# Fourier transform and two feed-forward layers: part of the fold on TensorE, and other sequences of GpSimd, ScalarE and the DMA queue

## What is computed

```python
X = np.fft.fft(np.fft.fft(x, axis=1), axis=2).real      # x: 2 x 3008 x 256
rms = sqrt(mean(X*X, -1) + 1e-6);  xn = X / rms * rms_g
h = silu(xn @ w_gate) * (xn @ w_val) @ w_out            # d_ff 1536
out = (h2 * cos(h2)) @ w2_out,   h2 = h @ w_in          # d_ff 2048
```

## Time and profile before

| | us |
|---|---|
| median of 3 runs (1007.44 to 1008.67) | 1007.55 |
| the profiled execution: its time | 1008.31 |
| its span | 1006.5 |
| PE busy in the span | 985.5 (98%) |
| DVE busy | 752.1 (75%) |
| ACT busy | 636.7 (63%) |
| POOL busy | 366.1 (36%) |

### The profile page before, as it was taken

How to read it: one execution, slowest core, us unless ns; L and a number is a source line. 1 busy time by engine, 2 the same in 40 slices (tenths; PEclk the granted TensorE clock), 3 DMA queues, 4 the chain that set the end, 5 groups by cost and what they waited for, 6 DMA issues and landing times.

```text
span 1006.5 us, 12914 instructions
## 1 busy us (share of the span) xinstructions
PE 985.5 (98%) x4464; PEld 815.2 (81%) x4464; DVE 752.1 (75%) x1028; ACT 636.7 (63%) x804; POOL 366.1 (36%) x303
## 2 busy tenths in 40 slices
PE   8878999999999999999999999999999999999998
PEld 7766888888888888888888888888888888888886
DVE  6576998767887767887767887677887676887665
ACT  3455667876348776447776437876437876547777
POOL 0266988104771004771003772003762002761000
PEclk9989999999999999999999999999999999999999
DMA  9822210000000000001000101000100000100001
GB/s 323 287 79 78 79 32 1 10 1 39 3 24 18 1 1 15 27 5 36 0 0 0 41 0 41 0 0 1 41 0 31 0 0 0 41 0 0 0 0 41
DMA packets 10416, 32.67 MB, mean 32 GB/s; under 512 B 2376, under 2 KB 6344, under 8 KB 9736
## 3 DMA queue, kind: packets, MB, share of 16 engines
q1 hardware_dynamic: 10308, 32.22, 9.2%
q10 hardware_dynamic: 68, 0.01, 0.0%
HBM read 22.95 MB, written 9.26 MB: 32 GB/s over the span
## 4 chain that ended last, share of the span: by engine, by line
PE 93%; issue 2%; ACT 1%; POOL 1%; DVE 1%; DMA 0%; ACTq 0%; SPq 0%; DVEq 0%; POOLq 0%
PE ps L474 30%; PE ps L476 29%; PE ps L475 29%; PE ps L418 1%; PE ps L433 1%; PE ps L450 1%; POOL work L1091 1%; PE ps L448 1%; DMA x_sb<-x 0%; PE ps L462 0%; PE ps L404 0%; ACT uv L587 0%; DVE pq L822 0%; POOL dif_lo L989 0%; POOL sum_lo L989 0%
## 5 line engine op out<-in xcount | busy, mean ns | idle before, releaser
L474 PE MATMUL ps<-h_hi,wo_hi 128*128 128x502 f32 x672 | 261.9, 390 | 1.9 <-DVE h_lo L873 1.8
L476 PE MATMUL ps<-h_hi,wo_lo 128*128 128x502 f32 x672 | 261.4, 389 | 0.0
L475 PE MATMUL ps<-h_lo,wo_hi 128*128 128x502 f32 x672 | 261.2, 389 | 0.0
L989 POOL TENSOR_TENSOR h_lo<-work,h_hi 128x502 fp32r<-128x502 f32 x92 | 101.7, 1113 | 373.1 <-ACT h_hi L701 372.5
L686 ACT ACTIVATE h_hi<-work 128x502 fp32r<-128x502 f32 x132 | 82.6, 626 | 185.5 <-POOL work L1091 184.6
L976 DVE SCALAR_TENSOR_TENSOR work<-work,ps 128x1004 f32<-128x1004 f32 (+1 forms) x109 | 117.2, 1075 | 95.3 <-ACT work L778 94.7
L962 DVE SCALAR_TENSOR_TENSOR work<-work,ps 128x1004 f32<-128x1004 f32 (+1 forms) x109 | 116.5, 1074 | 48.6 <-ACT work L764 48.6
L474 PEld LDWEIGHTS ps<-h_hi,wo_hi 128*128 128x128 f32 x672 | 126.2, 188 | 30.4 <-issue 2.8
L474 PE MATMUL ps<-x_hi,win_hi 128*128 128x502 f32 x384 | 149.9, 390 | 0.0
L475 PE MATMUL ps<-x_lo,win_hi 128*128 128x502 f32 x384 | 149.3, 389 | 0.0
L476 PE MATMUL ps<-x_hi,win_lo 128*128 128x502 f32 x384 | 149.2, 388 | 0.0
(11 more groups left out here) (87 smaller groups left out, 1388.5 us busy)
## 6 DMA issues: line engine op xcount, KB each, us to landing
out<-y_sb SPq DMA_DIRECT2D x10, 502.0 KB, 3.0
x_sb<-x SPq DMA_DIRECT2D x6, 768.0 KB, 10.5
uv_t<-uv_dram SPq DMA_DIRECT2D x6, 502.0 KB, 3.5
win_raw<-win SPq DMA_DIRECT2D x1, 2048.0 KB, 19.9
wo_raw<-wo SPq DMA_DIRECT2D x1, 2048.0 KB, 8.6
raw_b<-w1b SPq DMA_DIRECT2D x1, 1536.0 KB, 20.1
wo_raw<-wo SPq DMA_DIRECT2D x1, 1536.0 KB, 23.2
raw_a<-w1a SPq DMA_DIRECT2D x1, 1536.0 KB, 25.3
```

The costliest lines, as they stand in the source:

```text
L474: nc.tensor.matmul(acc, w_hi, v_hi, start=start, stop=False)
L475: nc.tensor.matmul(acc, w_hi, v_lo, start=False, stop=False)
L476: return nc.tensor.matmul(acc, w_lo, v_hi, start=False, stop=stop)
L989: nc.gpsimd.tensor_tensor(dst, src, hi.bitcast(F32), ALU.subtract).then_inc(s, 1)
```

## The change

- **Fold.** `seq1` is twice as wide and holds its negative too. For the chunks 3, 5, 7 and 9 DVE runs the sum alone (L800), and PE makes sum and difference of the two halves by accumulation: two products where there was one. From chunk 4 on one `warm_up` product stands ahead of a chunk in place of two. The tables for column 0 are changed to suit.
- **Slots.** Four buffers of squares in place of two, in the region of `x_sb`; eight rows of means in place of four.
- **Steps.** `RMS_AT`, `SCALE_AT`, `MIX_AT`, `W1_HI_AT` and `WO1_AT` have other steps, `mean_copy` has a list of its own, `split_uv(0)` is at p = 13 (before: 12), `root(1)` at 14, epsilon and reciprocal of group 1 at steps 29 and 32.
- **DMAs.** `raw_a` is loaded ahead of the second part of `seq2` and of `wo1`; SP issues the spreading of all means but the first two; the load of `win2` and the second store of `uv` come later.
- **POOL's list.** Squares first; `inverse(0)` ahead of the `wo1` parts; three `wo1` parts in the steps and three in tile 0 (before: four and two); `inverse(1)` in tile 0 after block 3.

```diff
--- before.py
+++ after.py
...
+HALF_FOLDED = (3, 5, 7, 9)
...
+    seq1 = seq1.reshape(P, -1)
+    seq1 = np.concatenate([seq1, -seq1], axis=1)
...
+    odd = np.arange(P + 1) % 2
+    feat[0, :P + 1] = 1 - odd
...
-    feat[:, FEAT:FEAT + P + 1] = (-1.0) ** np.arange(P + 1)
+    feat[:, FEAT:FEAT + P + 1] = odd
...
-    return {"t_seq1": f(seq1.reshape(P, -1), 2 * BATCH * 2 * K1), "t_feat": f(feat, FEAT + DIM),
+    return {"t_seq1": f(seq1, 4 * BATCH * 2 * K1), "t_feat": f(feat, FEAT + DIM),
...
-        squares = sb("squares", [2, 2, MEAN_COLS], o_o2h)
-        ROWS = 4
-        mean_row = sb("mean_row", [ROWS, MEAN_COLS], o_o2h + pad(16 * MEAN_COLS))[0:1, :, :]
-        assert o_o2h + (16 + 4 * ROWS) * MEAN_COLS + 32 <= o_o2l
+        SQUARES, ROWS = 4, 8
+        squares = sb("squares", [SQUARES, 2, MEAN_COLS], o_i2h)
+        mean_row = sb("mean_row", [ROWS, MEAN_COLS], o_o2h)[0:1, :, :]
+        assert 8 * SQUARES * MEAN_COLS <= WI2B and 4 * ROWS * MEAN_COLS <= WO2B
...
-        seq1 = sb("seq1", [2 * BATCH * 2 * K1], o_h + UVB)
-        assert UVB + 16 * BATCH * K1 <= 4 * TA
+        seq1 = sb("seq1", [4 * BATCH * 2 * K1], o_h + UVB)
+        assert UVB + 32 * BATCH * K1 <= 4 * TA
...
+        def half_folded(m):
+            return any(CHUNK_AT[i] <= m < CHUNK_AT[i + 1] for i in HALF_FOLDED)
...
-        RMS_AT = [8, 10, 14, 18, 22, 26, 30]
+        RMS_AT = [8, 10, 15, 20, 23, 27, 32]
+        MEAN_COPY_AT = [2, 3, 7, 9, 11, 13, 15]
+        ACT_MEANS = 2
...
         def rms_bank(q):
...
         def means_copied(p):
-            return [q for q, at in enumerate(RMS_AT) if (at - 2) // 2 == p]
+            return [q for q, at in enumerate(MEAN_COPY_AT) if at == p]
...
         def bank_pair(q):
...
-        SCALE_AT = [5, 6, 7, 8, 9, 10]
-        MIX_AT = [13, 14, 16, 17, 19, 20, 22, 23, 25, 26, 29, 31]
-        W1_HI_AT = [7, 9, 11, 13, 15, 16]
-        WO1_AT = [4, 5, 5, 6]
-        WO1_EARLY = len(WO1_AT)
+        SCALE_AT = [4, 5, 6, 7, 10, 13]
+        MIX_AT = [8, 9, 11, 12, 14, 15, 17, 18, 20, 21, 23, 24]
+        W1_HI_AT = [5, 7, 9, 11, 13, 15]
+        WO1_AT = [6, 8, 10, 12]
+        WO1_EARLY, WO1_LO_EARLY = len(WO1_AT), 3
...
-        SEQ2_FIRST = 8
+        SEQ2_FIRST = 10
...
+            load(raw_a[:, :], w1a, raw_a_in)
...
-            load(raw_a[:, :], w1a, raw_a_in)
-            sp.wait_ge(n1_done, 2 * NG)
-            load(win2_raw[:, :], win2, win2_in)
+            def spread_mean(q):
+                a, z = part_cols(q)
+                sp.wait_ge(mean_out, q + 1)
+                sp.dma_start(stat[stat_rows(*PART_ROWS[q]), 0, :], mean_row[:, q % ROWS, 0:z - a]
+                             ).then_inc(mean_in[q], 16)
...
             def store_inv(b, rows, at):
...
-            store_uv(0, (slice(FIRST_ROWS, K1 - 1), slice(K1 - 1, K1)))
+            spread_mean(2)
...
+            spread_mean(3)
+            store_uv(0, (slice(FIRST_ROWS, K1 - 1), slice(K1 - 1, K1)))
+            spread_mean(4)
+            load(win2_raw[:, :], win2, win2_in)
...
-            sp.wait_ge(inv_done, 2)
-            store_inv(0, (slice(FIRST_ROWS, K1 - 1), slice(K1 - 1, K1)), sum(TAKE[:FIRST_ROWS]))
...
-                sp.wait_ge(mean_in[q], 16)
+                spread_mean(q)
...
+            sp.wait_ge(inv_done, 2)
+            store_inv(0, (slice(FIRST_ROWS, K1 - 1), slice(K1 - 1, K1)), sum(TAKE[:FIRST_ROWS]))
...
             def store_y(t):
...
-                                warm_up(2)
+                                warm_up(2 if CHUNK_AT.index(m) < 4 else 1)
...
-                        last = nc.tensor.matmul(
-                            ps[:, (2 * g + c) % 4, i * COLS1:(i + 1) * COLS1],
-                            x_sb[:, m * XM + c * P:m * XM + (c + 1) * P], seq1[:, :],
-                            start=True, stop=True)
+                        acc = ps[:, (2 * g + c) % 4, i * COLS1:(i + 1) * COLS1]
+                        even, odd = (x_sb[:, m * XM + r * P:m * XM + (r + 1) * P] for r in range(2))
+                        if half_folded(m):
+                            nc.tensor.matmul(acc, even, seq1[:, 0:COLS1], start=True, stop=False)
+                            last = nc.tensor.matmul(acc, odd, seq1[:, c * COLS1:(c + 1) * COLS1],
+                                                    start=False, stop=True)
+                        else:
+                            last = nc.tensor.matmul(acc, odd if c else even, seq1[:, 0:COLS1],
+                                                    start=True, stop=True)
...
-                nc.tensor.matmul(ps[0:1, rms_bank(q), 0:z - a], mean_w, squares[:, q % 2, 0, 0:z - a],
+                nc.tensor.matmul(ps[0:1, rms_bank(q), 0:z - a], mean_w, squares[:, q % SQUARES, 0, 0:z - a],
...
             def square(q):
...
-                if q >= 2:
-                    act.wait_ge(ms_done, q - 1)
+                if q >= SQUARES:
+                    act.wait_ge(ms_done, q - SQUARES + 1)
...
-                nc.scalar.activation(squares[:, q % 2, :, 0:z - a], uv[PART_ROWS[q][0]][:, :, a:z],
+                nc.scalar.activation(squares[:, q % SQUARES, :, 0:z - a], uv[PART_ROWS[q][0]][:, :, a:z],
...
             def mean_copy(q):
...
-                act.wait_ge(mean_out, q + 1)
-                act.dma_start(stat[stat_rows(*PART_ROWS[q]), 0, :], mean_row[:, q % ROWS, 0:z - a]
-                              ).then_inc(mean_in[q], 16)
+                if q < ACT_MEANS:
+                    act.wait_ge(mean_out, q + 1)
+                    act.dma_start(stat[stat_rows(*PART_ROWS[q]), 0, :], mean_row[:, q % ROWS, 0:z - a]
+                                  ).then_inc(mean_in[q], 16)
...
             def root(group):
...
+                if p == 14:
+                    root(1)
...
-                    root(1)
-                if p == 12:
...
-                    if first and i == 2:
+                    if first and i == 1:
...
             for i in range(XL):
...
-                one, other = part[:, :, 1:P], part[:, :, P + 1:DIM]
-                nc.vector.tensor_tensor(part[:, :, 0:DIM], part[:, :, 0:DIM], part[:, :, DIM:XM], ALU.add
-                                        ).then_inc(even_done, 1)
-                dve.wait_ge(even_done, i + 1)
+                one, other = part[:, :, 0:P], part[:, :, P:DIM]
+                last = nc.vector.tensor_tensor(part[:, :, 0:DIM], part[:, :, 0:DIM], part[:, :, DIM:XM], ALU.add)
+                if i in HALF_FOLDED:
+                    last.then_inc(folded, 1)
+                    continue
+                last.then_inc(even_done, 1)
+                full = i + 1 - sum(k < i for k in HALF_FOLDED)
+                dve.wait_ge(even_done, full)
...
-                dve.wait_ge(odd_done, i + 1)
+                dve.wait_ge(odd_done, full)
...
-                if G == 27:
+                if G == 29:
...
-                if G == 30:
+                if G == 32:
...
             def lo1(t, i, g):
...
             def add_squares(q):
...
-                part = squares[:, q % 2, :, 0:z - a]
+                part = squares[:, q % SQUARES, :, 0:z - a]
...
-            add_squares(0)
-            add_squares(1)
-            wo1_part(0)
-            add_squares(2)
-            wo1_part(1)
-            wo1_part(2)
-            add_squares(3)
-            wo1_part(3)
-            inverse(0)
+            for q in range(3):
+                add_squares(q)
...
-            add_squares(4)
+            add_squares(3)
+            inverse(0)
+            wo1_part(0)
...
+            add_squares(4)
+            wo1_part(1)
...
+            wo1_part(2)
+            add_squares(6)
...
-            add_squares(6)
...
+            add_squares(7)
...
-            add_squares(7)
-            pool.wait_ge(sq_added, 8)
-            inverse(1)
-            pool.wait_ge(inv_done, 2)
...
             def wo2_part(k):
...
-                    if first and 6 <= i < 8:
-                        wo1_part(WO1_EARLY + i - 6)
+                    if first and i == 3:
+                        pool.wait_ge(w1_lo_done, W1_EARLY + 4)
+                        inverse(1)
+                        pool.wait_ge(inv_done, 2)
+                    if first and 5 <= i < 8:
+                        wo1_part(WO1_LO_EARLY + i - 5)
...
```

## The result

Seven runs of the changed kernel have a median of 1005.3 us (1004.9 to 1006.33), seven of the kernel before 1008.27 (1007.44 to 1009.75): a ratio of 0.9971, with a 95% interval of 0.9960 to 0.9983. So it is faster, as forecast, but by 3 us where I forecast 13, and 1005.3 lies above the range of 989.5 to 1003. The profiled execution took 1005.34 us for a span of 1003.6.

The account below looks back on a forecast made before the run. PE was taken to bound the six tiles from the first `down` on (911.3 us, not shortened); 2.75 - 15.8 - 1.65 + 1.4 = -13.3 gave a span of 993.2, forecast as 995.0 us, range 989.5 to 1003.

Parts of the forecast that it names:

- The fold, +2.75: Stretch up to the first feature product: PE's doubled products bind, so steps begin at 28.9 in place of 26.15.
- rival (b): Fold: bound by DVE after all, so 2.75 turns into -2 and the total is 990.2; chance 0.12.
- The head, -1.65: From `up1` to the first `down` of tile 0: 1.65 us less, with bounds 0.5 and 1.76.
- Tile 0, +1.4: Tile 0: `inverse(1)` adds about 0.4 us and the `wo1` rest at block 5 about 1.0; bounds 0 and 3.
- The steps, -15.8: Stretch from the first feature product to the first `up1`: 40.5 us in place of 56.35.
- My wait of 1.1 us: Steps: PE waits 1.1 us at step 23 for squares 4, expected at 56.0 behind `inverse(0)` and three weight rests.
- The cover of "1 to 2.5 us": Steps: time between POOL's adding of squares and PE's need, which would go if POOL were stretched.
- rival (a): Steps: one or two mixes held through a whole POOL run, 4.1 us each, total 999 to 1003; chance 0.20.
- (c): Steps 17 to 24: four or more mixes held at 4.1 us each, slower than before, 1011; chance 0.04.
- (d): Steps: POOL's late squares only move to other reductions, four waits of 3.0 us with half clock, 1007; chance 0.04.
- the reductions' 1 us: Sign in the changed profile: PE's waits on reductions of squares come to 1 us in all.
- `up1` at 69.5: Sign in the changed profile: the steps end and the first `up1` product of tile 0 starts at 69.5 us.

Follow-up runs that it names:

- experiment 3: The kernel before with squares 4 and a wait for the eighth mix ahead of the first `w1` rests in POOL's list: 1008.33 us, ratio 0.9992.
- experiment 7: The kernel before with one wait of POOL for its own first Newton step, right behind that step: 1008.71 us, ratio 0.9992.
- experiment 11: The changed kernel with POOL's wait behind the Newton step and the last six mixes three steps later: 999.01 us, ratio 0.9905.
- experiment 1: The changed kernel with the whole fold on DVE again and two warm-up products ahead of each chunk: 1003.51 us, ratio 0.9937.
- experiment 9: The changed kernel, half fold kept, with POOL's wait behind the Newton step and squares 4 and 5 earlier in its list: 997.09 us, ratio 0.9888.
- experiment 5: The changed kernel with one wait of POOL for its own first Newton step, ahead of the weight rests: 1002.28 us, ratio 0.9930.
- experiment 4: Probe without the reference: one two-input DVE instruction started beside six gapless POOL subtractions of 128x512; it took 0.63 to 1.71 us in all 72 trials.
- experiment 12: Probe without the reference: one POOL subtraction, 1.25 us alone, begun among six DVE mixes in a row, with or without memsets between; 1.29 to 1.96 us.

## Why the prediction was right and wrong

**What bounds the kernel, and the sign: right.** From the first `down` on nothing was won; the whole gain lies ahead of it.

**The fold, +2.75, measured +3.44: right in its mechanism.** The last DVE instruction on `x_sb` began at 22.10, PE was busy with the products until the steps; so rival (b), the fold bound by DVE, is out. From chunk 3's warm-ups at 14.06 to the first features PE took 15.53 us, where I counted 28.9 - 13.05 = 15.85. The term was 0.7 too small because chunk 3 began 1.0 us later than in the earlier trace rows. That was no doing of the change: the load of the second chunk of `x` landed 5.7 us after its issue, and in the trace behind my rows 4.5. In the kernel before of experiments 3 and 7 it took 5.8 and 5.7. DVE's first instruction on that chunk in the kernel before of my rows, in the changed kernel and in experiment 7:

```profile
6.19 0.69 DVE L800 TENSOR_TENSOR x_sb<-x_sb 128x512 f32<-128x512 f32 x1 [1.43 <-DMA x_sb<-x]
...
7.43 0.69 DVE L825 TENSOR_TENSOR x_sb<-x_sb 128x512 f32<-128x512 f32 x1 [2.90 <-DMA x_sb<-x]
...
7.41 0.69 DVE L800 TENSOR_TENSOR x_sb<-x_sb 128x512 f32<-128x512 f32 x1 [2.62 <-DMA x_sb<-x]
```

PE's products came down to their short time later, too. With the late landing the kernel before reached its first feature product at 26.55 and 26.66, not at 26.15. So 0.4 to 0.5 of the 3.44 us lie in the one trace that I took as the base; in experiment 11, where the chunk landed after 4.9 us, the product came at 28.92. The runs put the price of the half fold at 1.9 to 3.0 us (2.4 where it is made in experiment 1, 1.9 in the profiles and 2.8 to 3.0 in the medians of experiment 9): DVE was relieved where it did not bind, and PE loaded where it does.

**The head, -1.65, measured -1.74: right.** The wait of 1.76 us in the earlier trace rows is gone.

**Tile 0, +1.4, measured +2.3: right in kind.** Of the rest two waits on `h_lo` can be seen, 0.54 at 124.05 and 0.59 at 130.41, where I had put them between blocks 4 and 6. The remaining 1.2 us lie in slips too small for the list of waits, and I have not tested them.

**The steps, -15.8, measured -6.95: wrong.** The runs divide the 49.40 - 40.5 = 8.9 us. The hold: 49.40 - 45.89 = 3.5 (experiment 5). Squares 4 behind three weight rests, with the half clock: 45.89 - 41.05 = 4.8 (experiment 9). Left: 0.55. Two steps of the prediction failed.

The first is the one that gave POOL's instructions the durations of the old trace. Squares 3 ended at 52.07 where I had 48.7. Of the 3.4 us of delay 0.7 is the fold, 2.1 the length of the instruction (2.97 instead of 0.85), 0.6 the rests ahead of it (1.81 and 1.72). The Newton step took 2.9 instead of 2.3 us; the three rests behind it took 3.7, less than the 4.3 I had given them, since the held mix left POOL alone. So squares 4 were there 3.3 us late, and PE at them only 1.3. My wait of 1.1 us became 3.3, and that carried me over the line that I had drawn myself: "no wait of PE is longer than 1.1 us; half clock followed waits of 2 us and more". (That line is no sure one: in experiment 3 waits of 2.80 and 3.11 us had the clock at 1.00 behind them, and only the one of 4.68 had 0.50.) The cover of "1 to 2.5 us" was named, but no case was made of its loss. Without the two mixes beside them squares 3 had their 0.84 us again (experiment 11); POOL's times under mixes stood in the earlier trace rows as 1.25 to 1.5 us, which was too kind a sample. A case in which squares 4 come 3 us late should have been among those of the forecast.

The second is rival (a), "One or two mixes are held through a whole POOL run". It came true, once, and with 4.1 us for it I was near the 3.5 measured in the steps, though the mix took 10.54 us. Its time of 999 came out six microseconds low because the late squares came on top (4.8), and fold and tile 0 (1.6). The error was the chance of 0.20, and the reason: "For it: the unbroken run" is what experiment 4 refutes, so that the rival came true for another reason than the one I gave. That 4.1 lies near 3.5 is in part luck, as it is the price of the old hold of 6.32 us. The old trace had one such hold, at the one place where a run followed a Newton step; the same step with a longer run behind it and more mixes beside was in the new list. "Against: one hold in the old trace" counted the mixes; it should have asked what was special about that one. I kept it a rival because "all other mixes under 1.4" had POOL busy beside them too; now we know that they had no narrow instruction ahead of them.

**Rivals (c) and (d).** No four holds, so (c) did not come. Of (d), squares that are late at another reduction, there was one instance, 3.3 us in place of four at 3.0. (Its 1007 is four waits alone; with the half clock that it names, 2 us each as in (a), it would have been 1015.) The result is a mixture of (a) and a part of (d), to which no case of mine belonged: they were taken as exclusive, and they share one cause, POOL's stretched list. Experiments 3 and 7 say the same of the old kernel: its hold could be taken away at no gain, because squares came late behind it.

**What would show it.** Of the signs named beforehand, the feature product (28.9, measured 29.59), the last DVE instruction on `x_sb` (before 23) and the `down` without a wait held; the reductions' 1 us, `up1` at 69.5, "no mix over 2 us" and the clock failed. With the half fold and the cures of experiment 9 they hold as well: steps of 41.05 us for 40.5, and a first `down` at 81.52 for 80.5. So the walk of the new lists was sound for an undisturbed POOL.

## What to carry to other kernels

When a walk of a new list says that an engine is ready one or two microseconds ahead, stretch that engine's durations by the worst row of each kind beside the other engine's work, and see whether a wait grows to the size of those behind which the clock fell in the old trace: here the place of two POOL instructions was worth 4.8 us, a wait and the half clock behind it. An outlier in the old trace (one mix of 6.32 us) is to be explained by what stood just ahead of it, before the change moves it; removing it is worth something only if nothing behind it is late. And put work on the engine that has slack in that stretch: accumulating the sum on TensorE freed VectorE where it had time and cost 2 to 3 us. And look at the start of more than one execution before taking a base from it: between executions of the kernel before, with one DMA landing earlier or later, the first stretch differed by 0.5 us here.

## What the hardware showed that I had not expected

**A narrow GpSimd instruction shuts VectorE out.** After a GpSimd instruction on 6 partitions without a wait behind it, a VectorE instruction with two SBUF inputs was kept out until GpSimd came to a stand: in 48 of 48 trials, 5.25 to 6.59 us in place of 0.63 to 1.71, and 10.54 us in the changed kernel. A wait of GpSimd for its own narrow instruction ends it: 24 of 24 trials, and 3 us of the kernel for one line (experiment 5). The Trainium skill, SBUF — State Buffer, section Who interferes with whom, lets the first to come keep the shared ports for its whole instruction. Sixty of the 72 trials of the plain probe agree. In the other 12 the VectorE instruction began 0.04 to 0.22 us behind the start of GpSimd's and was not held, so the order of the starts in the profile does not always tell who has the ports; and the narrow trials go beyond the rule. A reason can be had from the GPSIMD Engine Reference of the Trainium skill, section Instruction dispatch: each of the eight cores works on 16 partitions of its own and starts the next instruction as soon as it is through with its own share. Then a subtraction on 6 partitions occupies one core, the other seven run ahead, and some core is always in the midst of an instruction, so that the ports are never free. That is a reading of mine that fits all the trials; no run here looks at single cores, so the cause in the engine is argued, not shown.

**DVE stretches POOL as well.** A sum of squares of 0.84 us took 2.97 with two mixes beside it, 49.10 in the changed kernel against 48.44 in experiment 11. Both mixes, at 49.56 and 50.62, began within the sum and took 0.73, no longer than alone. A row of six mixes cost a POOL instruction 0.7 us at most (experiment 12), but in experiment 11 one mix beside a rest cost it 0.83 (2.10 in place of 1.27), and two of these would make 1.7 of the 2.1. How one POOL instruction comes to be interrupted twice, and the rest of the 2.1, no run here shows. Copies of `pq` and the end of the reciprocal on 6 partitions ran beside the sum in experiment 11 as well, and it took 0.84. What stays open is a narrow VectorE instruction shortly ahead of mixes, which was not tried.
